# The last 18 tiles of layer 2: two T2 products of three on GpSimd, and every second v = b2|h| + b1 on ScalarE

## The chip, the cores and the metric

The kernel runs on one core of a Trainium2 chip. The metric is the device time of one launch in microseconds (us). The core has a matrix engine (TensorE, PE in the profile), a vector engine (VectorE, DVE), a scalar engine (ScalarE, ACT), a general engine (GpSimd, POOL) and a queue engine (SyncE, SP). Each takes its own instructions in order and waits for the others through semaphores.

## The reference

An attention stage is followed by two layers of the form "tokens times w_in, a function of each element, times w_out". There are 12288 tokens of width 128, and the hidden width is 2048. The function of the second layer is a rational one, and it is the part that the change touches:

```
h  = x @ w_in
P  = a0 + a1*h + a2*h^2 + a3*h^3
Q  = 1 + |b0|*|h| + |b1|*h^2
out = (P / (Q + 1e-6)) @ w_out
```

## The kernel before

**Tiles.** The tokens are cut into 24 chunks of 512 and the hidden width into 16 blocks of 128. One tile is one block of one chunk, 128 x 512 numbers in f32, and there are NB = 384 tiles per layer. The two layers run together in one loop over steps s: step s does tile s of layer 1 and tile t = s - 19 of layer 2 (LAG = 19). Layer 1 ends with s = 383, so that the last tiles of layer 2, from t = 366 on (OFF0 = NB - 18), run with no work of layer 1 beside them. In the text a tile of this stage is named by k = t - 366, from 0 to 17.

**One tile of layer 2.** TensorE writes h into PSUM (`in2`). ScalarE writes u = |h| (L550) and t1 = a3*h + a2 (L551, the scale in a register, the bias from a tile). GpSimd writes v = b2*u + b1 (L404) and w = v*u (L412); here b1 and b2 are the two absolute coefficients in the tile `babs`. T2 = t1*h is made by VectorE (L776, L747), or by GpSimd (L410). GpSimd is given SBUF tiles only, so for a T2 of its own ScalarE first copies h into `hcb` (L557). VectorE makes T3 = (T2 + a1)*h (L770). ScalarE makes ln(1 + w) (L568) and from it r = 1/Q by an exponential (L584), written over h. VectorE makes y = (T3 + a0)*r (L761), the correction e from w and r (L790), and the result g = (e - 2)*y (L785). TensorE adds g times w_out to the sum of the chunk (`out2`, L944 in the last chunk).

**Order.** The order on each engine is written out by hand. In the last stage ScalarE takes for tile t: u, t1, the copy of h if GpSimd makes this T2, then ln and the exponential of tile t-1. GpSimd takes v, T2 if it is its own, and w, all of tile t. VectorE takes y of t-2, T3 of t-1, T2 of t if it is its own, g of t-3, e of t-2. In the last stage TensorE runs three matmuls per tile whose result is not used (L982). When a chunk ends, ScalarE also copies the finished sum out (L514); this happens once in the stage, ahead of tile k = 6. Ahead of tile k = 1 it splits the last chunk's input (L526, L528), and GpSimd makes the low part of it (L397).

**Who makes T2.** `by_pool(t)` says whether GpSimd makes T2 of tile t: of the last 18 tiles every odd k, nine of them; before that, one tile of 16. `pool_t2(t)` counts these tiles. The semaphore `v_rdy` counts the v's.

**The register.** Between the attention stage and the layers ScalarE waits for the last attention sum and loads a3 into a register (L505); after that it takes the first tile of layer 1 (L578, L541). `babs` is written by VectorE (L694).

Of the kernel before, what the change touches and what calls it, by code (L numbers as in the profile page):

```python
# [22 lines left out]
ALU = mybir.AluOpType  # L23
ACT = mybir.ActivationFunctionType
# [6 lines left out]
def build_program(nc, qT, kvT, w_sr, w_in1, w_out1, w_in2, w_out2, coef_a, coef_b, outT):  # L31
# [11 lines left out]
    NF = DFF // P  # L43
    SA = 2 * TPC
    ITERS = NCH // 2
    NB = NCH * NF
# [5 lines left out]
    OFF0 = NB - 18  # L52
    HC_RING = 2
    H1_RING, H2_RING = 2, 4
    U_RING, W_RING, LN_RING, T_RING, R_RING, G_RING = 3, 4, 2, 6, 4, 4
# [11 lines left out]
    with ExitStack() as ctx:  # L67
# [22 lines left out]
        ca, cb, babs = sb("ca", [P, 4], F32), sb("cb", [P, 2], F32), sb("babs", [P, 2], F32)  # L90
# [44 lines left out]
        def sem(name):  # L135
            return ctx.enter_context(nc.semaphore(name))
# [22 lines left out]
        sqh_rdy, sql_rdy = sem("sqh_rdy"), sem("sql_rdy")  # L159
        x2f_rdy, x2l0_rdy = sem("x2f_rdy"), sem("x2l0_rdy")  # L160
        wo1h_rdy, wo1_rdy, g1h_rdy, g1l_rdy = map(sem, ("wo1h_rdy", "wo1_rdy", "g1h_rdy", "g1l_rdy"))
        hc_rdy, t2p_rdy = sem("hc_rdy"), sem("t2p_rdy")
        o_out = [sem("o_out0"), sem("o_out1")]
        wout1_in = sem("wout1_in")
# [4 lines left out]
        def need(eng, s, value):  # L169

            if not isinstance(value, int) or value > 0:
                eng.wait_ge(s, value)
# [58 lines left out]
        T2_COL = 7  # L231

        def by_pool(t):

            return t % 2 == 1 if OFF0 <= t < NB else 0 <= t < OFF0 and t % NF == T2_COL

        POOL_T2 = [t for t in range(NB) if by_pool(t)]

# [48 lines left out]
        def _(pool):  # L287
# [100 lines left out]
            for s in range(STEPS):  # L388
                if s % NF == 5 and 1 <= s // NF < NCH - 1:
                    x1_high(s // NF + 1)  # L390
                    x1_low(s // NF + 1)
                t = s - 3
                if chunk_end(t) and t > NF:
                    c = t // NF
                    pool.wait_ge(x2h_rdy, c + 1)
                    pool.wait_ge(x2f_rdy, c)
                    nc.gpsimd.tensor_tensor(x2l[:, c % 2, :], x2f[:, c % 2, :], x2h[:, c % 2, :].bitcast(F32),  # L397
                                            ALU.subtract).then_inc(x2_rdy, 1)
                t = s - LAG
                if in_b(t):  # L400
                    w = wb[:, t % W_RING, :]
                    u = ub[:, t % U_RING, :]
                    pool.wait_ge(u_rdy, t + 1)
                    nc.gpsimd.tensor_scalar(w, u, babs[:, 1:2], babs[:, 0:1], ALU.mult, ALU.add).then_inc(v_rdy, 1)  # L404
                    if by_pool(t):
                        n = pool_t2(t)
                        p = tb[:, t % T_RING, :]
                        pool.wait_ge(t1_rdy, t + 1)
                        pool.wait_ge(hc_rdy, n + 1)
                        nc.gpsimd.tensor_tensor(p, p, hcb[:, n % HC_RING, :], ALU.mult).then_inc(t2p_rdy, 1)  # L410
                    pool.wait_ge(v_rdy, t + 1)
                    nc.gpsimd.tensor_tensor(w, w, u, ALU.mult).then_inc(w_rdy, 1)  # L412
                t = s
                if in_b(t) and not on_act(t):
                    r = r1[:, t % R_RING, :]
                    pool.wait_ge(r1_rdy, t + 1)
                    need(pool, g1_used, t - G_RING + 1)
                    nc.gpsimd.tensor_tensor(g1[:, t % G_RING, :], r, r, ALU.mult).then_inc(sqp_rdy, 1)  # L418
                    if halved(t):
                        n = halves(t)  # L420
                        pool.wait_ge(sqh_rdy, n + 1)
                        pool.wait_ge(sqp_rdy, squares_pool(t))
                        nc.gpsimd.tensor_tensor(g1l[:, n % 2, :], g1[:, t % G_RING, :], g1h[:, n % 2, :].bitcast(F32),
                                                ALU.subtract).then_inc(sql_rdy, 1)
# [3 lines left out]
        def _(act):  # L428
# [74 lines left out]
            act.wait_ge(coef_in, 32)  # L503
            a3 = act.alloc_register("a3")
            nc.scalar.reg_load(a3, ca[0:1, 3:4].bitcast(mybir.dt.int32))  # L505

            for s in range(STEPS):
                t = s - LAG - 5
                if chunk_end(t):
                    c = t // NF  # L510
                    need(act, o_out[c % 2], c // 2 * 16)
                    if c < NCH - 1:
                        act.wait_ge(g2_used, t + 1)
                        nc.scalar.activation(osb[:, c % 2, :], ACC2, ACT.Copy, scale=-1.0).then_inc(o_rdy, 1)  # L514
                    else:
                        for h in range(2):
                            act.wait_ge(g2_used, 2 * (t + 1) - (NB - NF) - 1 + h)
                            nc.scalar.activation(osb[:, c % 2, h * HT:(h + 1) * HT], ACC_END[h], ACT.Copy,
                                                 scale=-1.0).then_inc(o_rdy, 1)

                t = s - 3
                if chunk_end(t) and t > NF:
                    c = t // NF
                    act.wait_ge(g1_used, t + 1)
                    need(act, h2_rdy, (c - 1) * NF)
                    nc.scalar.activation(x2h[:, c % 2, :], ACC1, ACT.Identity).then_inc(x2h_rdy, 1)  # L526
                    need(act, x2_rdy, c - 2)
                    nc.scalar.activation(x2f[:, c % 2, :], ACC1, ACT.Identity).then_inc(x2f_rdy, 1)  # L528

                t = s - 1  # L530
                if halved(t):
                    n = halves(t)
                    act.wait_ge(r1_rdy, t + 1)
                    need(act, g1_used, t - G_RING + 1)
                    nc.scalar.activation(g1h[:, n % 2, :], r1[:, t % R_RING, :], ACT.Square).then_inc(sqh_rdy, 1)

                t = s - 1
                if in_b(t) and on_act(t) and s != LAG:
                    act.wait_ge(r1_rdy, t + 1)
                    need(act, g1_used, t - G_RING + 1)  # L540
                    nc.scalar.activation(g1[:, t % G_RING, :], r1[:, t % R_RING, :], ACT.Square).then_inc(sqa_rdy, 1)  # L541

                if s == NF + 1:
                    act.wait_ge(g1_used, NF)
                    nc.scalar.activation(x2h[:, 0, :], ACC1, ACT.Identity).then_inc(x2h_rdy, 1)

                t = s - LAG
                if in_b(t):
                    act.wait_ge(h2_rdy, t + 1)
                    nc.scalar.activation(ub[:, t % U_RING, :], h2(t), ACT.Abs).then_inc(u_rdy, 1)  # L550
                    nc.scalar.activation(tb[:, t % T_RING, :], h2(t), ACT.Identity,  # L551
                                         bias=ca[:, 2:3],
                                         scale=a3).then_inc(t1_rdy, 1)
                    if by_pool(t):
                        n = pool_t2(t)
                        need(act, t2p_rdy, n + 1 - HC_RING)
                        nc.scalar.activation(hcb[:, n % HC_RING, :], h2(t), ACT.Identity).then_inc(hc_rdy, 1)  # L557

                t = s - 1
                if in_b(t) and on_act(t) and s == LAG:  # L560
                    act.wait_ge(r1_rdy, t + 1)
                    need(act, g1_used, t - G_RING + 1)
                    nc.scalar.activation(g1[:, t % G_RING, :], r1[:, t % R_RING, :], ACT.Square).then_inc(sqa_rdy, 1)

                t = s - LAG - 1
                if in_b(t):
                    act.wait_ge(w_rdy, t + 1)
                    nc.scalar.activation(lnb[:, t % LN_RING, :], wb[:, t % W_RING, :], ACT.Ln,  # L568
                                         bias=Q_ONE).then_inc(ln_rdy, 1)

                t = s
                if in_b(t):
                    act.wait_ge(h1_rdy, t + 1)
                    if t < NF + R_RING:
                        need(act, g1h_rdy, min(t - R_RING + 1, NF))
                    elif not on_act(t - R_RING):
                        act.wait_ge(sqp_rdy, squares_pool(t - R_RING))
                    nc.scalar.activation(r1[:, t % R_RING, :], H1[t % H1_RING], ACT.Relu).then_inc(r1_rdy, 1)  # L578

                t = s - LAG - 1  # L580
                if in_b(t):
                    act.wait_ge(t3_rdy, t + 1)
                    act.wait_ge(ln_rdy, t + 1)
                    nc.scalar.activation(h2(t), lnb[:, t % LN_RING, :], ACT.Exp,  # L584
                                         scale=-1.0).then_inc(r_rdy, 1)
# [441 lines left out]
```

## Time and profile before

| | |
|---|---|
| median of 3 runs | 1517.66 us (1517.64 to 1517.86) |
| the profiled execution's own time | 1517.89 us |
| its span, first to last instruction | 1515.9 us |
| busy share PE, DVE, ACT, POOL | 98%, 95%, 91%, 82% |
| granted TensorE clock | 1.000 over the span |

The busy shares are means over the whole run. The stage that the change touches is the last 4% of it, from about 1455 us to the end. There, in one slice of 5.62 us after another, the profile repeats the same pair of tiles.

### The profile page before, as it was taken

To read this page: it belongs to the slowest core of one execution; us is meant where nothing else is said; L and a number is where in the kernel's file an instruction comes from. 1 tells how busy PE (TensorE), PEld (TensorE's weight loads), DVE (VectorE), ACT (ScalarE), POOL (GpSimd) and SP (SyncE) were. 2 spreads that over 40 slices of the span, in tenths; PEclk is the share of its full clock that TensorE was granted. 3 is DMA by queue.
4 is the path that set the end of the run, shared out by engine and by line. 5 is a ranking of instruction groups with operands and counts; after the bars stand their busy time and mean duration, and the time that the engine had idled before them with its cause. 6 is when DMAs were issued, how large, how long until landed. Compare 5 with 4: busy or idle time off the path is not lost.

```text
span 1515.9 us, 20584 instructions
## 1 busy us (share of the span) xinstructions
PE 1483.7 (98%) x5576; PEld 991.1 (65%) x5576; DVE 1445.2 (95%) x2549; ACT 1378.8 (91%) x2672; POOL 1248.3 (82%) x1225
## 2 busy tenths in 40 slices
PE   5999999999999999999999999999999999999988
PEld 4999999765666666666666666666666666666655
DVE  7888888889999999999999999999999999999998
ACT  3777777689999999999999999999999999999997
POOL 4544445359999999999999999999999999999897
PEclk9999999999999999999999999999999999999999
DMA  6200001000000000000000000000000000000000
GB/s 224 84 21 28 21 27 43 1 1 1 8 8 8 1 8 8 8 8 1 7 8 8 0 8 8 8 1 8 7 8 1 8 8 8 8 1 8 8 8 7
DMA packets 11518, 24.21 MB, mean 16 GB/s; under 512 B 1440, under 2 KB 2336, under 8 KB 11168
## 3 DMA queue, kind: packets, MB, share of 16 engines
q1 hardware_dynamic: 11424, 23.14, 4.5%
q8 instruction: 36, 0.59, 0.2%
q14 instruction: 58, 0.48, 0.1%
HBM read 16.85 MB, written 6.29 MB: 15 GB/s over the span
## 4 chain that ended last, share of the span: by engine, by line
PE 88%; DVE 5%; ACT 2%; POOL 2%; issue 1%; DMA 1%; SPq 0%; POOLq 0%; ACTq 0%; DVEq 0%
PE psum L937 19%; PE psum L974 18%; PE psum L801 11%; PE psum L800 11%; PE psum L802 11%; PE psum L889 6%; PE psum L852 6%; PE psum L874 4%; DVE tb L727 1%; DVE tb L736 1%; DVE tb L753 1%; DVE g1h L713 1%; DVE psum L741 1%; POOL tb L410 1%; DMA X<-kvT 1%
## 5 line engine op out<-in xcount | busy, mean ns | idle before, releaser
L412 POOL TENSOR_TENSOR wb<-wb,ub 128x512 f32<-128x512 f32 x384 | 496.4, 1293 | 29.4
L937 PE MATMUL psum<-tb,wout 128*128 128x512 f32 x736 | 375.8, 592 | 2.5 <-DVE tb L785 2.3
L974 PE MATMUL psum<-g,wout 128*128 128x512 f32 x690 | 352.4, 592 | 0.2 <-ACT x2f L528 0.2
L404 POOL TENSOR_SCALAR wb<-ub,babs 128x512 f32<-128x512 f32 x384 | 296.0, 771 | 35.5 <-ACT ub L550 30.3
L800 PE MATMUL psum<-x2h,win2h 128*128 128x512 f32 x384 | 283.3, 738 | 2.6 <-POOL x2l L397 2.5
L727 DVE SCALAR_TENSOR_TENSOR tb<-tb,ca,psum 128x512 f32<-128x512 f32 x364 | 267.8, 736 | 4.6 <-ACT psum L584 4.5
L736 DVE SCALAR_TENSOR_TENSOR tb<-tb,ca,psum 128x512 f32<-128x512 f32 x365 | 269.6, 739 | 0.0
L551 ACT ACTIVATE tb<-psum,ca 128x512 f32<-128x512 f32 x384 | 267.1, 696 | 0.0
L550 ACT ACTIVATE ub<-psum 128x512 f32<-128x512 f32 x384 | 233.0, 607 | 23.5 <-PE psum L802 23.5
L568 ACT ACTIVATE lnb<-wb 128x512 f32<-128x512 f32 x384 | 248.3, 647 | 5.2 <-POOL wb L412 4.8
L753 DVE SCALAR_TENSOR_TENSOR tb<-psum,tb 128x512 f32<-128x512 f32 x364 | 248.1, 682 | 2.6
L741 DVE SCALAR_TENSOR_TENSOR psum<-wb,psum 128x512 f32<-128x512 f32 x364 | 249.5, 685 | 0.0
L584 ACT ACTIVATE psum<-lnb 128x512 f32<-128x512 f32 x384 | 240.1, 625 | 2.6 <-DVE tb L770 0.6
L974 PEld LDWEIGHTS psum<-g,wout 128*128 128x128 f32 x690 | 130.9, 190 | 163.7 <-issue 162.0
L578 ACT ACTIVATE r<-psum 128x512 f32<-128x512 f32 x384 | 234.9, 612 | 2.4 <-PE psum L802 0.3
L747 DVE TENSOR_TENSOR tb<-tb,psum 128x512 f32<-128x512 f32 x343 | 232.5, 678 | 4.0 <-ACT tb L551 4.0
L418 POOL TENSOR_TENSOR g<-r 128x512 f32<-128x512 f32 x184 | 191.9, 1043 | 33.2 <-ACT r L578 33.2
L334 POOL TENSOR_SCALAR pnorm<-prob,stat 128x768 f32<-128x768 f32 x96 | 87.3, 909 | 127.8 <-DVE stat L637 122.0
L937 PEld LDWEIGHTS psum<-tb,wout 128*128 128x128 f32 x736 | 138.4, 188 | 36.4 <-DVE tb L785 3.8
L801 PE MATMUL psum<-x1l,win1h 128*128 128x512 f32 x384 | 153.0, 398 | 0.0
L801 PE MATMUL psum<-x2l,win2h 128*128 128x512 f32 x384 | 152.9, 398 | 0.0
L800 PE MATMUL psum<-x1h,win1h 128*128 128x512 f32 x384 | 151.9, 396 | 0.0
(109 smaller groups left out, 2506.6 us busy)
## 6 DMA issues: line engine op xcount, KB each, us to landing
qraw<-qT SPq DMA_DIRECT2D x23, 256.0 KB, 2.6
outT<-osb SPq DMA_DIRECT2D x23, 256.0 KB, 2.0
X<-kvT SPq DMA_DIRECT2D x15, 384.0 KB, 7.7
wraw<-w_in SPq DMA_DIRECT2D x2, 1024.0 KB, 8.3
X<-kvT SPq DMA_DIRECT2D x2, 192.0 KB, 10.5
outT<-osb SPq DMA_DIRECT2D x2, 128.0 KB, 1.8
qraw<-qT SPq DMA_DIRECT2D x1, 192.0 KB, 10.2
wsr<-w_sr SPq DMA_DIRECT2D x1, 64.0 KB, 1.8
```

The source lines that it names most:

```text
L404: nc.gpsimd.tensor_scalar(w, u, babs[:, 1:2], babs[:, 0:1], ALU.mult, ALU.add).then_inc(v_rdy, 1)
L412: nc.gpsimd.tensor_tensor(w, w, u, ALU.mult).then_inc(w_rdy, 1)
L551: nc.scalar.activation(tb[:, t % T_RING, :], h2(t), ACT.Identity, bias=ca[:, 2:3], scale=a3).then_inc(t1_rdy, 1)
L568: nc.scalar.activation(lnb[:, t % LN_RING, :], wb[:, t % W_RING, :], ACT.Ln, bias=Q_ONE).then_inc(ln_rdy, 1)
L727: nc.vector.scalar_tensor_tensor(out=y, in0=y, scalar=ca[:, 0:1], in1=r, op0=ALU.add, op1=ALU.mult).then_inc(y_rdy, 1)
L736: nc.vector.scalar_tensor_tensor(out=p, in0=p, scalar=ca[:, 1:2], in1=h2(t), op0=ALU.add, op1=ALU.mult).then_inc(t3_rdy, 1)
L741: nc.vector.scalar_tensor_tensor(out=r, in0=wb[:, t % W_RING, :], scalar=Q_ONE, in1=r, op0=ALU.add, op1=ALU.mult).then_inc(e_rdy, 1)
L753: nc.vector.scalar_tensor_tensor(out=y, in0=h2(t), scalar=-2.0, in1=y, op0=ALU.add, op1=ALU.mult).then_inc(g2_rdy, 1)
L800: mm(out, lh, rh, start=start, stop=False)
L801: mm(out, lh, rl, start=False, stop=False)
L937: mm(ACC2, wout2[:, f, :], tb[:, t % T_RING, :], start=(f == 0), stop=(f == NF - 1))\
L974: mm(ACC1, wout1[:, f, :], g1[:, t % G_RING, :], start=(f == 0), stop=(f == NF - 1))\
```

## The change

Three things change, all within the last 18 tiles but for one register load. T2 is made by GpSimd for k = 1, 2, 4, 5, 7, 8, and so on, 12 tiles in place of 9. For every odd k, v is made by ScalarE (an Identity activation with scale b2 in a register and bias b1 from `babs`), right behind t1 and ahead of the copy of h; GpSimd's w then waits for that. And ScalarE loads b2 into a register beside a3, with a wait for `babs`.

```
         def by_pool(t):
-            return t % 2 == 1 if OFF0 <= t < NB else 0 <= t < OFF0 and t % NF == T2_COL
+            return (t - OFF0) % 3 > 0 if OFF0 <= t < NB else 0 <= t < OFF0 and t % NF == T2_COL
+        def v_on_act(t):
+            return OFF0 <= t < NB and (t - OFF0) % 2 == 1
+        def v_acts(t):
+            return sum(v_on_act(x) for x in range(t))
 ...  (GpSimd)
-                    pool.wait_ge(u_rdy, t + 1)
-                    nc.gpsimd.tensor_scalar(w, u, babs[:, 1:2], babs[:, 0:1], ALU.mult, ALU.add).then_inc(v_rdy, 1)
+                    if not v_on_act(t):
+                        pool.wait_ge(u_rdy, t + 1)
+                        nc.gpsimd.tensor_scalar(w, u, babs[:, 1:2], babs[:, 0:1], ALU.mult, ALU.add).then_inc(v_rdy, 1)
                     if by_pool(t):
                         ... T2 on GpSimd, unchanged
-                    pool.wait_ge(v_rdy, t + 1)
+                    if v_on_act(t):
+                        pool.wait_ge(va_rdy, v_acts(t) + 1)
+                    else:
+                        pool.wait_ge(v_rdy, t + 1 - v_acts(t))
                     nc.gpsimd.tensor_tensor(w, w, u, ALU.mult).then_inc(w_rdy, 1)
 ...  (ScalarE, before the loop)
+            act.wait_ge(babs_rdy, 1)
+            b2 = act.alloc_register("b2")
+            nc.scalar.reg_load(b2, babs[0:1, 1:2].bitcast(mybir.dt.int32))
 ...  (ScalarE, behind t1)
+                    if v_on_act(t):
+                        act.wait_ge(u_rdy, t + 1)
+                        need(act, e_rdy, t + 1 - W_RING)
+                        nc.scalar.activation(wb[:, t % W_RING, :], ub[:, t % U_RING, :], ACT.Identity,
+                                             bias=babs[:, 0:1], scale=b2).then_inc(va_rdy, 1)
```

## Rows read from the trace of the kernel before

**Rows 1.** Busy time in one pair of tiles: stretch, us, busy (x count) by engine, clock, DMA.
```profile
1486.93:1492.55 5.62, 5.04 (x21) 3.61 (x21) 5.62 (x10) 5.03 (x11) 5.32 (x6) 1.00 0.00 0
```

**Rows 2.** Chain that ended last, in one pair: start us, us, what.
```profile
1483.09 1.29 POOL tb L410
1484.38 1.26 POOL wb L412
...
1485.66 0.64 ACT lnb L568
```

**Rows 3.** Timeline of ScalarE, k = 9 and 10: start us, us, engine line op, [idle before].
```profile
1481.30 0.58 ACT L550 ACTIVATE ub<-psum 128x512 f32<-128x512 f32 x1
1481.78 0.68 ACT L551 ACTIVATE tb<-psum,ca 128x512 f32<-128x512 f32 x1
1482.35 0.60 ACT L557 ACTIVATE hcb<-psum 128x512 f32<-128x512 f32 x1
1482.82 0.64 ACT L568 ACTIVATE lnb<-wb 128x512 f32<-128x512 f32 x1
1483.56 0.60 ACT L584 ACTIVATE psum<-lnb 128x512 f32<-128x512 f32 x1
1484.09 0.58 ACT L550 ACTIVATE ub<-psum 128x512 f32<-128x512 f32 x1
1484.57 0.68 ACT L551 ACTIVATE tb<-psum,ca 128x512 f32<-128x512 f32 x1
1485.66 0.63 ACT L568 ACTIVATE lnb<-wb 128x512 f32<-128x512 f32 x1 [0.41 <-POOL wb L412]
```

**Rows 4.** Timeline of GpSimd, k = 1, then k = 9 and 10.
```profile
1459.50 0.78 POOL L404 TENSOR_SCALAR wb<-ub,babs 128x512 f32<-128x512 f32 x1
1460.23 1.29 POOL L410 TENSOR_TENSOR tb<-tb,hcb 128x512 f32<-128x512 f32 x1
...
1483.09 1.29 POOL L410 TENSOR_TENSOR tb<-tb,hcb 128x512 f32<-128x512 f32 x1 [0.23 <-ACT hcb L557]
1484.34 1.29 POOL L412 TENSOR_TENSOR wb<-wb,ub 128x512 f32<-128x512 f32 x1
1485.61 0.77 POOL L404 TENSOR_SCALAR wb<-ub,babs 128x512 f32<-128x512 f32 x1
1486.47 1.27 POOL L412 TENSOR_TENSOR wb<-wb,ub 128x512 f32<-128x512 f32 x1
```

**Rows 5.** Timeline of VectorE, T2 and g of k = 10 and 7.
```profile
1485.52 0.68 DVE L776 TENSOR_TENSOR tb<-tb,psum 128x512 f32<-128x512 f32 x1
1486.11 0.68 DVE L785 SCALAR_TENSOR_TENSOR tb<-psum,tb 128x512 f32<-128x512 f32 x1
```

**Rows 6.** Timeline of ScalarE, a square from SBUF to SBUF.
```profile
1442.02 0.64 ACT L541 ACTIVATE g<-r 128x512 f32<-128x512 f32 x1
1442.55 0.60 ACT L550 ACTIVATE ub<-psum 128x512 f32<-128x512 f32 x1
```

**Rows 7.** The line of the register load: duration ns min/median/max, first and last start us.
```profile
L505 ACTq TENSOR_LOAD <-ca x1: 465/465/465, 293.3 to 293.3; - x1
```

**Rows 8.** Timeline where layer 1 begins.
```profile
293.90 0.60 ACT L578 ACTIVATE r<-psum 128x512 f32<-128x512 f32 x1
...
296.10 0.47 PE L800 MATMUL psum<-g1h,wo1h 128*128 128x512 f32 x1 [0.59 <-DVE g1l L716]
```

**Rows 9.** Timeline of ScalarE: u of k = 1, copy out, u of k = 7 and 17, last ln.
```profile
1457.99 0.60 ACT L550 ACTIVATE ub<-psum 128x512 f32<-128x512 f32 x1
...
1472.46 0.58 ACT L514 ACTIVATE osb<-psum 128x512 f32<-128x512 f32 x1
...
1475.66 0.60 ACT L550 ACTIVATE ub<-psum 128x512 f32<-128x512 f32 x1 [0.32 <-PE psum L802]
...
1503.78 0.58 ACT L550 ACTIVATE ub<-psum 128x512 f32<-128x512 f32 x1
...
1508.12 0.63 ACT L568 ACTIVATE lnb<-wb 128x512 f32<-128x512 f32 x1 [1.49 <-POOL wb L412]
```

More of the change, by code:

```diff
@@ L161, in build_program @@
         wo1h_rdy, wo1_rdy, g1h_rdy, g1l_rdy = map(sem, ("wo1h_rdy", "wo1_rdy", "g1h_rdy", "g1l_rdy"))
+        va_rdy = sem("va_rdy")
         hc_rdy, t2p_rdy = sem("hc_rdy"), sem("t2p_rdy")
```

## The prediction, made before the result was known

> **What bounds the stage now.** I looked first at the busy time by stretches, because the shares of the page are means over a run in which the change touches only the last 60 us. In one pair of tiles (5.62 us) VectorE is busy all 5.62, GpSimd 5.32, ScalarE 5.03 and TensorE 5.04 [rows 1]. That says VectorE, but the shares hide how near the others are. So I read the chain of waits next, and it doesn't run through VectorE: it goes from GpSimd's T2 to w to ScalarE's ln [rows 2], and from there along ScalarE to the next copy of h. The reader is to see in the timelines that this loop closes. From ScalarE's copy of h to GpSimd's T2 is 1483.09 - 1482.35 = 0.74; from T2 to w 1.25; from w to ln 1485.66 - 1484.34 = 1.32 [rows 3, 4]. On ScalarE, start to start, u takes 0.48, t1 0.57, the copy 0.475, ln 0.73 (the exponential needs its result) and the exponential 0.54 [rows 3]. The loop is 0.74 + 1.25 + 1.32 + 0.73 + 0.54 + 0.48 + 0.57 = 5.63 per pair, which is what the pair takes. VectorE's work happens to be as long: two limits lie on each other, and a third is close. ScalarE's own work in a pair is 2 x 2.32 + 0.475 = 5.12, with 0.52 free (the trace shows 0.41 as idle, the rest is the tail of t1) [rows 3]. GpSimd's own free time is the 0.23 before its T2 [rows 4]. An edit here must be read as a loop over all engines.
>
> **What the change takes away.** VectorE loses 3 T2 of 0.60 each, start to start (1486.11 - 1485.52) [rows 5]: per six tiles its work goes from 3 x 5.62 = 16.9 to 16.3. GpSimd loses nine v and gains three T2: per six tiles it has 3 x 0.86 for v with w behind it or 0.73 with T2 behind it, 4 x 1.25 and 6 x 1.27, at most 15.2 instead of 16.9 [rows 4]. Both have room then, some 2.7 and 2.5 per tile.
>
> **What it adds, and where.** Everything else lands on ScalarE: nine v and three more copies of h. The copy is 0.475 [rows 3]. The v isn't in the trace. It reads SBUF and writes SBUF, as the square does, which takes 0.54 from start to start [rows 6]; and it has a bias from a tile and a scale in a register, as t1 has, which takes 0.57 where the plain copy from the same place takes 0.475 [rows 3]. So I take 0.54 + 0.09 = 0.63. Bounds: 0.475 below, as cheap as the copy, and 0.73 above, the spacing of ln, the longest that any activation of this stage shows [rows 3]. Its wait for u costs nothing: u ends 0.58 after its start, and v could start at 1.05 anyway. Its wait for e of tile t-4 is long over. What is queued behind v is the copy of h and with it GpSimd's T2 and w, so a late v delays both.
>
> The page "ScalarE: Activation LUTs" of the Trainium skill, section "What ACT_TABLE_LOAD costs", gives an activation with a pointer bias as 280 ns plus 0.833 ns per element, with neighbours overlapping by 93 ns; an estimate from it is 0.61 for v, and with it the sum below would be about 0.1 lower. No run here has shown v yet, but t1 in the trace, 0.68 busy, is a little under the 0.71 of that rule.
>
> The Trainium skill's page "GPSIMD Engine Reference", section "Engine selection", says that a product of two tiles belongs on VectorE, as GpSimd is about twice as slow with two inputs. The trace agrees (1.29 against 0.68), and going by this rule alone the three moved T2 would lose 3 x (1.25 - 0.60) = 2.0 us. By the loop they cost something else, which is worked out next.
>
> **The new cycle.** The pattern repeats every six tiles. I go along ScalarE's queue from one u to the next. A plain tile is 0.48 + 0.57 + 0.73 + 0.54 = 2.32; the copy adds 0.475, v adds 0.63.
> - k = 1, 5 (both): 2.32 + 0.475 + 0.63 = 3.43.
> - k = 4 (copy): 2.80.
> - k = 2 (copy): 2.80 of its own. Ln of k = 1 can't start before 0.74 + 1.25 + 1.32 = 3.31 after the copy of k = 1, and ScalarE arrives at 0.475 + 0.73 + 0.54 + 0.48 + 0.57 + 0.475 = 3.27: a stall of 0.04, so 2.83.
> - k = 3 (v): 2.95 of its own. GpSimd was still with w of k = 1 when u of k = 2 was there, so for k = 2 v, T2 and w come behind each other: from the copy of k = 1, T2 at 0.74, w at 1.99, v of k = 2 at 3.25, T2 at 3.98, w at 5.23, ln at 6.55. ScalarE arrives at 3.31 + 0.73 + 0.54 + 0.48 + 0.57 + 0.63 = 6.26. A stall of 0.29: 3.24.
> - k = 0 (nothing): 2.32 of its own, but ln of k = 5 needs 3.31 from the copy of k = 5 and ScalarE arrives at 2.80: 2.83.
>
> Together 2 x 3.43 + 2.80 + 2.83 + 3.24 + 2.83 = 18.56 for six tiles, against 3 x 5.62 = 16.87 before: +1.69, or 0.28 per tile. Of this 0.85 is ScalarE's own work beyond the old cycle (17.71 against 16.87), and the rest are three stalls in which GpSimd is late. VectorE needs 16.3 and waits. So the limit moves from a loop over GpSimd to ScalarE's queue, and the three T2 taken from VectorE buy nothing.
>
> **The whole stage.** k = 0 is untouched. From u of k = 1 at 1457.99 [rows 9] the steps 3.43, 2.83, 3.24, 2.80 and 3.43 bring ScalarE to the copy out at 1473.72 instead of 1472.46. From there TensorE sets the next distance: u of k = 7 waited for it and came 3.20 after the copy out [rows 9], so it comes at 1476.92 instead of 1475.66, +1.26 (the copy out and this wait hide the stall of k = 6). From k = 7 to 17 are ten steps: 3.43 + 2.83 + 3.24 + 2.80 + 3.43 + 2.83 + 3.43 + 2.83 + 3.24 + 2.80 = 30.86, before 1503.78 - 1475.66 = 28.12: +2.74. For k = 17, from u to the last ln, there are 0.48 + 0.57 + 0.63 + 0.74 + 1.25 + 1.32 = 4.99 instead of 4.34 [rows 9]: +0.65. What follows the last ln is the same. Sum 1.26 + 2.74 + 0.65 = 4.65 us.
>
> **The second register.** Loading a3 took 0.465 [rows 7], from 293.3 to 293.77, and the first tile of layer 1 started at 293.90, when TensorE's result was there: the first load is hidden. A second one behind it ends at about 294.27. Nothing covers it: VectorE waits for that tile, and TensorE waits 0.59 for VectorE [rows 8]; the chain of waits stays on this pair through the whole first chunk. The wait for `babs` itself is over. I take +0.45; bounds 0 (if TensorE or VectorE makes it up) and 0.55 (a load, a wait and a little dispatch).
>
> **Sum.** 1517.89 is the profiled execution's own time; 1517.89 + 4.65 + 0.45 = 1522.99. It stands 0.23 above the median of the runs, so I predict 1522.8. Six of the nine v count fully (those of k = 3, 9, 15 lie before a stall), so the bounds of v give 6 x (0.475 - 0.63) = -0.9 and 6 x (0.73 - 0.63) = +0.6; with the register the likeliest case spans 1521.4 to 1523.5.
>
> **Rivals.**
> - *Only ScalarE's work counts.* If GpSimd, with less to do on average, caught up wherever I see a stall, six tiles would take 17.71: +0.85 per six, 2.4 over the 17 tiles, with the register +2.8: 1520.5. For it: GpSimd has 1.7 us less work per six tiles. Against: the stalls come from latency (copy, T2, w, ln in line), not from load, and the 0.41 idle in front of ln [rows 3] is the same thing today. 9%.
> - *VectorE is the true limit, and the edit is a gain.* If the loop only looks closed and ScalarE's instructions can be packed tighter behind each other than they stand now, the time follows VectorE: -3 x 0.60, and +0.45: 1516.3. For it: VectorE's 5.62 of 5.62 [rows 1]. It decides where ScalarE's added work per pair, 0.63 + 0.16 for a third of a copy, fits into its free 0.52: v and the share of the copy would have to be under 0.52, thus v under 0.36. The shortest activation of this size in the rows is 0.475 apart. 4%.
> - *The T2 pairs fall out worse.* GpSimd's v of k = 2 waits for w, and if T2 behind it took 0.86 instead of 0.73 to follow, the stall of k = 3 grows by 0.13 and the total by 0.4; if v also came at its upper bound, 1523.9. 8%.
> - *The forecast:* 79%.
>
> **Chances.** What a measurement of this kernel can tell from no change is about 0.2%, 3.0 us: below 1514.6, or above 1520.7. The forecast and the third rival lie above; the first rival lies just inside. Faster 0.04, same 0.10, slower 0.86. The range reaches down to the first rival and up past the third: 1520.4 to 1524.3.
>
> **What would show it.** In the profile after: v as an activation of about 0.72 us, followed by the next after 0.63; a cycle of 18.56 us for six tiles, with ScalarE busy nearly throughout and idle only ahead of ln of k = 5, 11 (0.4 as the profile counts it) and of k = 2, 8, 14; VectorE waiting for the exponential where it had no gap; GpSimd no longer in the chain except at those places; two register loads, and the first tile of layer 1 at about 294.35. I am wrong if the cycle is under 17.7, if VectorE has no idle time, or if v takes under 0.5.

## The result

| | changed kernel | before |
|---|---|---|
| median of 7 runs each | 1522.77 us (1522.46 to 1524.05) | 1517.86 us (1517.64 to 1518.38) |
| the profiled execution's own time, span | 1522.46, 1520.5 | 1517.89, 1515.9 |

The ratio is 1.0034, with a 95% interval of 1.0023 to 1.0046: slower by 4.9 us, where 1522.8 was forecast. The runs of the changed kernel lie in two groups, four from 1522.46 to 1522.77 and three from 1523.66 to 1524.05. The forecast had the first group and not the second, and the median falls into the first by one run.

The page of the changed kernel shows where the work went. ScalarE has 12 activations more (2672 before), VectorE 3 and GpSimd 6 instructions less:

```profile
span 1520.5 us, 20600 instructions
...
PE 1485.9 (98%) x5576; PEld 992.3 (65%) x5576; DVE 1444.4 (95%) x2546; ACT 1385.4 (91%) x2684; POOL 1245.1 (82%) x1219
```

The busy time by stretches of the changed kernel (us, then TensorE, weight loads, VectorE, ScalarE, GpSimd, clock, DMA) has one cycle of six tiles, from u of k = 9 to u of k = 15, in its last row. It answers to the pair in [rows 1]:

```profile
1459.00:1460.00 1.00, 0.21 (x1) 0.21 (x2) 1.00 (x3) 1.00 (x3) 0.74 (x1) 0.98 0.00 0
1460.00:1462.00 2.00, 2.00 (x5) 1.21 (x5) 0.68 (x2) 1.91 (x4) 1.38 (x2) 0.50 0.03 8
1462.00:1464.00 2.00, 2.00 (x6) 1.11 (x5) 2.00 (x4) 1.91 (x5) 2.00 (x3) 0.66 0.00 0
...
1483.29:1501.77 18.48, 15.16 (x62) 10.85 (x61) 16.75 (x26) 17.30 (x33) 14.87 (x14) 1.00 0.00 0
```

Six tiles take 18.48 us in place of 16.87. VectorE, which had no gap, is free for 1.73 us of them and GpSimd for 3.61. ScalarE is now the busiest, with 1.18 us free in six tiles, 0.62 of it ahead of the two ln that wait for w (k = 8 and 11).

The first three rows show something else. TensorE has waited for x2l, the low part of the last chunk's input, and behind this wait its granted clock is 0.50 (1.2 GHz) for over 3 us. In the trace of before the same wait is as long and the clock behind it is 1.00. The timelines of TensorE, first in the changed kernel and then in the kernel before:

```profile
1459.79 0.67 PE L821 MATMUL psum<-x2h,win2h 128*128 128x512 f32 x1 [2.19 <-POOL x2l L406]
...
1474.49 1.13 PE L965 MATMUL psum<-tb,wout 128*128 128x256 f32 x4 [2.14 <-ACT osb L530]
```

```profile
1459.57 0.50 PE L800 MATMUL psum<-x2h,win2h 128*128 128x512 f32 x1 [2.19 <-POOL x2l L397]
...
1473.10 1.13 PE L944 MATMUL psum<-tb,wout 128*128 128x256 f32 x4 [0.98 <-ACT osb L514]
```

The second row of each is the wait for the copy out, which grew from 0.98 to 2.14 us: ScalarE reaches the copy out 1.40 us later than before. Behind it the clock is 1.00 in both of these executions (1474 to 1478 us).

ScalarE's timeline shows the stretches that the prediction walked through: the first tile of layer 1; u of k = 1; the copy out; u of k = 7 and 9; v of k = 9 and the ln behind it; u of k = 11, and the v and the copy of h with it; the ln of that tile; u of k = 15 and 17; the last ln.

```profile
294.12 0.60 ACT L599 ACTIVATE r<-psum 128x512 f32<-128x512 f32 x1 [0.31 <-PE psum L823]
...
1458.21 0.60 ACT L566 ACTIVATE ub<-psum 128x512 f32<-128x512 f32 x1
...
1473.86 0.58 ACT L530 ACTIVATE osb<-psum 128x512 f32<-128x512 f32 x1
...
1477.05 0.60 ACT L566 ACTIVATE ub<-psum 128x512 f32<-128x512 f32 x1 [0.34 <-PE psum L823]
...
1483.29 0.58 ACT L566 ACTIVATE ub<-psum 128x512 f32<-128x512 f32 x1
...
1484.34 0.72 ACT L573 ACTIVATE wb<-ub,babs 128x512 f32<-128x512 f32 x1
1485.28 0.63 ACT L589 ACTIVATE lnb<-wb 128x512 f32<-128x512 f32 x1 [0.22 <-POOL wb L425]
...
1489.33 0.58 ACT L566 ACTIVATE ub<-psum 128x512 f32<-128x512 f32 x1
...
1490.38 0.72 ACT L573 ACTIVATE wb<-ub,babs 128x512 f32<-128x512 f32 x1
1490.99 0.59 ACT L578 ACTIVATE hcb<-psum 128x512 f32<-128x512 f32 x1
...
1494.29 0.63 ACT L589 ACTIVATE lnb<-wb 128x512 f32<-128x512 f32 x1 [0.40 <-POOL wb L425]
...
1501.77 0.58 ACT L566 ACTIVATE ub<-psum 128x512 f32<-128x512 f32 x1
...
1507.82 0.58 ACT L566 ACTIVATE ub<-psum 128x512 f32<-128x512 f32 x1
...
1512.75 0.63 ACT L589 ACTIVATE lnb<-wb 128x512 f32<-128x512 f32 x1 [1.47 <-POOL wb L425]
```

Who waited for whom from 1480 to 1509 us (us, times, longest): VectorE's y for the exponential, seven times, and ScalarE's ln for w only three times.

```profile
DVE tb L782 <- ACT psum L605: 2.7, 7, 0.8
...
ACT lnb L589 <- POOL wb L425: 0.8, 3, 0.4
```

The second register load is in the trace, shorter than the first (ns, start us):

```profile
L518 ACTq TENSOR_LOAD <-ca x1: 457/457/457, 293.3 to 293.3; - x1
...
L521 ACTq TENSOR_LOAD <-babs x1: 278/278/278, 293.8 to 293.8; - x1
```

The profile puts the 0.31 of idle time ahead of the first tile (294.12) down to TensorE. But the matmul that it names was over at about 293.88, and the second load ran until about 294.1, so the tile more likely waited for the load:

```profile
293.49 0.39 PE L823 MATMUL psum<-x1h,win1l 128*128 128x512 f32 x1
```

### The profile page after: what moved, and what is told of

It reads as the page before. It is cut to its first block, busy times and chain, and to the rows that moved or that the text cites. A ratio compares the mean times of both kernels' runs of the same rounds, so it can differ in the third digit from the quotient of the medians.

```text
span 1520.5 us, 20600 instructions
## 1 busy us (share of the span) xinstructions
PE 1485.9 (98%) x5576; PEld 992.3 (65%) x5576; DVE 1444.4 (95%) x2546; ACT 1385.4 (91%) x2684; POOL 1245.1 (82%) x1219
## 2 busy tenths in 40 slices
DMA packets 11518, 24.21 MB, mean 16 GB/s; under 512 B 1440, under 2 KB 2336, under 8 KB 11168
## 4 chain that ended last, share of the span: by engine, by line
PE 88%; DVE 5%; ACT 3%; POOL 2%; issue 1%; DMA 0%; SPq 0%; POOLq 0%; ACTq 0%; DVEq 0%
PE psum L958 19%; PE psum L995 18%; PE psum L822 11%; PE psum L821 11%; PE psum L823 11%; PE psum L910 6%; PE psum L873 6%; PE psum L895 4%; DVE tb L748 1%; DVE tb L757 1%; DVE tb L774 1%; DVE g1h L734 1%; DVE psum L762 1%; POOL tb L420 1%; POOL wb L425 1%
## 5 line engine op out<-in xcount | busy, mean ns | idle before, releaser
L414 POOL TENSOR_SCALAR wb<-ub,babs 128x512 f32<-128x512 f32 x375 | 289.1, 771 | 37.3 <-ACT ub L566 32.5
```

## The experiments

All were run beside the kernel before on the same chip; its median there was 1517.87, 1517.90 and 1517.81 us in the three sets of four. In what was written ahead of them, "loops and queues" is the prediction's way of counting: each engine in its order, each wait with its latency.

| kernel | median (lowest to highest), us | against before | runs |
|---|---|---|---|
| reg_only | 1517.80 (1517.39 to 1518.22) | -0.1 | 11 |
| t2_only | 1520.29 (1520.00 to 1522.01) | +2.4 | 11 |
| v_only | 1523.19 (1523.08 to 1523.48) | +5.3 | 5 |
| v_late | 1521.59 (1520.60 to 1522.22) | +3.7 | 10 |
| reg_early | 1523.49 (1522.23 to 1524.46) | +5.6 | 5 |
| gap_filled | 1524.43 (1522.85 to 1524.66) | +6.5 | 5 |
| v_even | 1518.77 (1518.41 to 1519.30) | +0.9 | 11 |
| t2_trim | 1518.16 (1517.41 to 1518.61) | +0.3 | 11 |
| after_filled | 1523.27 (1523.02 to 1523.42) | +5.5 | 5 |
| before_filled | 1518.04 (1517.79 to 1518.40) | +0.2 | 11 |
| t2_skip1 | 1517.31 (1517.01 to 1517.73) | -0.5 | 11 |
| skip1_filled | 1518.16 (1517.50 to 1518.45) | +0.4 | 11 |

**One part at a time: t2_only.** The kernel before with only this line:

```
-            return t % 2 == 1 if OFF0 <= t < NB else ...
+            return (t - OFF0) % 3 > 0 if OFF0 <= t < NB else ...
```

> Only the 12 T2 on GpSimd, every v stays there. Theory A (loop through GpSimd): three tiles need at least 0.86 + 2 x 0.73 for v, 2 x 1.25 for T2 and 3 x 1.27 for w = 8.6 us on GpSimd alone, and some 8.8 with the wait for the copy, against 8.44 before: the stage is 2.2 us longer. Theory B (VectorE is the limit): 3 x 0.60 = 1.8 us shorter.

+2.4 us, theory A. GpSimd's timeline from v of k = 9 to v of k = 12 shows three tiles in 1494.08 - 1485.23 = 8.85 us, where 8.8 was expected, with one wait of 0.22:

```profile
1485.23 0.76 POOL L404 TENSOR_SCALAR wb<-ub,babs 128x512 f32<-128x512 f32 x1
...
1488.32 1.27 POOL L410 TENSOR_TENSOR tb<-tb,hcb 128x512 f32<-128x512 f32 x1 [0.22 <-ACT hcb L557]
...
1491.56 1.29 POOL L410 TENSOR_TENSOR tb<-tb,hcb 128x512 f32<-128x512 f32 x1
1492.80 1.31 POOL L412 TENSOR_TENSOR wb<-wb,ub 128x512 f32<-128x512 f32 x1
1494.08 0.78 POOL L404 TENSOR_SCALAR wb<-ub,babs 128x512 f32<-128x512 f32 x1
```

Three T2 taken from VectorE save nothing, although VectorE was busy all the time. In this kernel the loop's limit is GpSimd itself, whose own work is 8.6 of the 8.85. Four of its eleven runs, 1521.3 to 1522.0, stand apart from the rest, as in the changed kernel. The profiled execution (1521.52) is one of these four. In it TensorE waits for the copy out, the clock behind this wait is 0.71 from 1474 to 1476 us and 0.50 from 1476 to 1478, and ScalarE waits for h of k = 7. The rows of TensorE's and of ScalarE's timeline:

```profile
1473.87 1.17 PE L944 MATMUL psum<-tb,wout 128*128 128x256 f32 x4 [1.84 <-ACT osb L514]
```

```profile
1477.64 0.60 ACT L550 ACTIVATE ub<-psum 128x512 f32<-128x512 f32 x1 [1.11 <-PE psum L802]
```

**The other part: v_only.** The changed kernel with the old `by_pool`.

```
-            return (t - OFF0) % 3 > 0 if OFF0 <= t < NB else ...
+            return t % 2 == 1 if OFF0 <= t < NB else ...
```

> T2 stays at every odd k; v of every odd k is on ScalarE, ahead of the copy of h, with the register. Theory A (the v stands in the loop copy, T2, w, ln, exponential, u, t1): the pair takes 5.63 + 0.61 = 6.24 us, the stage is 5.0 longer, with the register +5.2, so more than the whole change. Theory B (ScalarE's work counts alone): the pair takes 5.12 + 0.61 = 5.73, the stage is 1.0 longer, with the register +1.2.

+5.3 us, theory A: one half of the change alone costs more than the whole. ScalarE's timeline in this kernel, from one ln that waits for w to the next:

```profile
1482.69 0.63 ACT L589 ACTIVATE lnb<-wb 128x512 f32<-128x512 f32 x1 [0.40 <-POOL wb L425]
...
1484.99 0.73 ACT L573 ACTIVATE wb<-ub,babs 128x512 f32<-128x512 f32 x1
1485.61 0.60 ACT L578 ACTIVATE hcb<-psum 128x512 f32<-128x512 f32 x1
...
1488.91 0.63 ACT L589 ACTIVATE lnb<-wb 128x512 f32<-128x512 f32 x1 [0.40 <-POOL wb L425]
```

The pair takes 6.22 us, the loop's 5.63 and v's 0.61, and the 0.40 of idle time in front of ln is where it was before: ScalarE isn't full, v simply stands in the loop. A low clock has a small share in the +5.3: from 1466 to 1468 us it is 0.50 in this trace, ScalarE waits 0.65 for h there, and that pair takes 6.45.

**The same instructions in other places: v_late and v_even.** In v_late the whole change stands, with the two blocks swapped:

```
+                    if by_pool(t):
+                        n = pool_t2(t)
+                        need(act, t2p_rdy, n + 1 - HC_RING)
+                        nc.scalar.activation(hcb[:, n % HC_RING, :], h2(t), ACT.Identity).then_inc(hc_rdy, 1)
                     if v_on_act(t):
...
-                    if by_pool(t):
...
```

> The whole change, but v is issued behind the copy of h and not ahead of it. No instruction is added or removed. Theory A: the v leaves the path copy, T2, w, and is done before w needs it; tiles with both cost what ScalarE needs, the stalls shrink: 2.1 us less than the change, +2.4 to +2.6 against the kernel before. Theory B (only the sum of ScalarE's work counts): no difference from the change, +4.6 to +5.

Its ten runs lie in two groups, four from 1520.60 to 1520.81 and six from 1521.46 to 1522.22. The lower one is 2.8 us above before and some 1.9 below the lower group of the change; expected were 2.4 to 2.6 and 2.1. The upper group, 1521.77 in the middle, is 1.9 below the upper group of the change (1523.70). The median of all ten, +3.7, falls into the upper group and is above what was expected. So order alone takes about two of the five microseconds. The busy time by stretches says what is left: ScalarE is busy 19.44 of 20 us.

```profile
1480.00:1500.00 20.00, 16.88 (x68) 11.93 (x66) 18.65 (x30) 19.44 (x36) 17.20 (x16) 1.00 0.00 0
```

v_even keeps the old T2 and makes v on ScalarE for k = 2, 4, 6 and so on (eight tiles), which have no copy of h:

```
-            return (t - OFF0) % 3 > 0 if OFF0 <= t < NB else ...
+            return t % 2 == 1 if OFF0 <= t < NB else ...
...
-            return OFF0 <= t < NB and (t - OFF0) % 2 == 1
+            return OFF0 < t < NB and (t - OFF0) % 2 == 0
```

> T2 stays at every odd k; v goes to ScalarE for the even k, which have no copy of h. Theory A (loops and queues): from the copy of an odd tile ScalarE needs 0.475 + 0.73 + 0.54 + 0.48 + 0.57 + 0.61 = 3.41 to the ln that GpSimd lets go after 3.31, so v fills the 0.50 in which ScalarE stood idle: 5.73 per pair, 0.9 us more over the stage, with the register +1.1. Against v at the odd tiles (+5.3 measured) the place of the same instruction decides over 4 us. Theory B (nine v on ScalarE cost the same wherever they stand): +5.

+0.9 us, theory A. In ScalarE's timeline v of k = 10 fills what was the stall: the ln behind it has no idle time, and the pair takes 1487.84 - 1482.13 = 5.71.

```profile
1482.13 0.58 ACT L566 ACTIVATE ub<-psum 128x512 f32<-128x512 f32 x1
...
1485.97 0.72 ACT L573 ACTIVATE wb<-ub,babs 128x512 f32<-128x512 f32 x1
1486.59 0.62 ACT L589 ACTIVATE lnb<-wb 128x512 f32<-128x512 f32 x1
...
1487.84 0.58 ACT L566 ACTIVATE ub<-psum 128x512 f32<-128x512 f32 x1
```

Eight v here cost 0.9 us, nine at the odd tiles 5.3. The 0.9 by itself isn't clear of the scatter (the interval of the ratio is 0.9997 to 1.0015), but the +5 of theory B is excluded.

**The register: reg_only and reg_early.** reg_only adds the wait and the load to the kernel before.

```
             nc.scalar.reg_load(a3, ca[0:1, 3:4].bitcast(mybir.dt.int32))
+            act.wait_ge(babs_rdy, 1)
+            b2 = act.alloc_register("b2")
+            nc.scalar.reg_load(b2, babs[0:1, 1:2].bitcast(mybir.dt.int32))
```

> Only the second register load (with its wait for babs) is added to the kernel before. Theory A (queue order and latency decide): its trace shows the first tile of layer 1 0.22 us later and all behind it with it, so +0.2 us, and the TensorE clock stays at 1.00 in every run, as it does before. Theory B (the prediction's own size): +0.45. Theory C (the shift of the start is what makes the TensorE clock drop behind the wait for x2l, seen in the changed kernel): most runs below clock 1.000, and some of them 1.2 us longer.

It measures less than it meant to: its trace has one register load, that of a3. Nothing uses b2 in this kernel and the program came out without the load, so only the wait can have run, and it has no cost that the runs resolve (the interval is 0.9991 to 1.0009). So neither the +0.2 nor the +0.45 was tested by this run, and theory C wasn't either. reg_early has both loads ahead of the last attention copy:

```
-            for j in range(TAIL_A):
+            for j in range(TAIL_A - 1):
                 step_a(ITERS, j)
-            act.wait_ge(pv_rdy, NCH)
-            act.wait_ge(ql_rdy, NCH)
             act.wait_ge(coef_in, 32)
             a3 = act.alloc_register("a3")
 ...  (both loads, unchanged)
+            step_a(ITERS, TAIL_A - 1)
+            act.wait_ge(pv_rdy, NCH)
+            act.wait_ge(ql_rdy, NCH)
```

> The whole change, but both register loads stand ahead of ScalarE's last attention copy, where it waits for TensorE anyway. Theory A (the second load, 0.278 us in the trace, delays the first tile of layer 1 by 0.20): that tile comes 0.70 after the copy again, as before, and the time is 0.2 us below the change's. Theory B (something else of the new program moved the start): no difference.

The loads now run at 288.6 and 289.1 us. The first tile of layer 1 comes 0.78 after the copy, with TensorE named as what it waited for; in the changed kernel it came 0.90 after it, before 0.70. Theory A expected 0.70, so 0.12 of the 0.20 came back. The lowest runs are 1522.23 and 1522.75, against 1522.46 for the change, so what this gives in the time lies within the scatter of the runs, and three of five are in the upper group. In the profiled execution, one of these three (1523.50), the place of the loss can be seen. TensorE's timeline, ScalarE's timeline and the stretches:

```profile
1474.19 1.30 PE L966 MATMUL psum<-tb,wout 128*128 128x256 f32 x4 [2.14 <-ACT osb L531]
...
1476.56 0.63 PE L822 MATMUL psum<-x2h,win2h 128*128 128x512 f32 x1
```

```profile
1478.08 0.60 ACT L567 ACTIVATE ub<-psum 128x512 f32<-128x512 f32 x1 [1.67 <-PE psum L824]
```

```profile
1474.00:1476.00 2.00, 1.81 (x6) 1.56 (x7) 1.83 (x4) 1.91 (x5) 1.92 (x3) 0.75 0.35 131
1476.00:1478.00 2.00, 2.00 (x6) 1.54 (x6) 2.00 (x4) 0.41 (x1) 1.17 (x1) 0.50 0.00 0
```

TensorE has stood for 2.14 us waiting for the copy out, the clock falls to 1.2 GHz, and the matmuls of h take 0.63 in place of 0.39. Just there, at k = 7, ScalarE waits for h: 1.67 us in place of the 0.34 of the changed kernel's profiled execution. That is 1.3 us, about the distance between the groups. In that other execution the clock fell at 1460 us, where ScalarE didn't wait for h, and it is one of the lower group.

**TensorE kept busy: gap_filled, after_filled, before_filled.** gap_filled is the changed kernel with 8 matmuls whose result isn't used:

```
+            def fill_gap():
+                pe.wait_ge(r1_rdy, NB)
+                for _ in range(8):
+                    mm(H1[1], win1h[:, 0:P], x1h[:, 0, :], start=True, stop=True)
 ...
+                if s == NB + 2:
+                    fill_gap()
```

> The whole change, and 8 matmuls whose result is not used are put on TensorE where it stands idle for 2.19 us waiting for x2l. Theory A (this idle time is what lets the TensorE clock fall to half, in a part of the runs, and costs up to 1.3 us there): the clock is 1.00 around 1460 us, and all runs lie together near 1522.5. Theory B (the clock falls because TensorE has more idle time in the whole stage): the runs still lie in two groups 1.2 us apart.

Theory A as written is refuted. The wait for x2l shrank from 2.19 to 0.34 (the eight stand one tile early and held up u of k = 1 by 0.31 too), but the low clock came later instead, in two places of the profiled execution, and three runs are at 1524.4 or above:

```profile
1464.00:1466.00 2.00, 2.00 (x5) 1.11 (x5) 1.80 (x3) 1.93 (x4) 2.00 (x3) 0.67 0.00 0
1466.00:1468.00 2.00, 2.00 (x6) 1.57 (x5) 1.96 (x5) 1.67 (x4) 1.80 (x2) 0.50 0.00 0
1474.00:1476.00 2.00, 1.21 (x3) 1.03 (x4) 1.57 (x3) 2.00 (x5) 2.00 (x3) 0.73 0.20 75
1476.00:1478.00 2.00, 2.00 (x6) 1.54 (x6) 2.00 (x4) 0.92 (x2) 1.69 (x2) 0.50 0.15 56
```

The first of these falls stands behind another wait of TensorE, 1.90 for VectorE's g:

```profile
1463.96 1.38 PE L958 MATMUL psum<-tb,wout 128*128 128x512 f32 x2 [1.90 <-DVE tb L806]
```

The second one stands behind the copy out again, after 2.20 us of waiting, and ScalarE waits 1.96 for h of k = 7. It isn't one gap, then. after_filled fills the stage: the same 8, 4 ahead of the first sum of the last chunk, and 4 per tile in place of 3, from two tiles earlier on. before_filled is the kernel before with the same edit.

```
-    WARM, WARM_B = 4, 3
+    WARM, WARM_B = 4, 4
...
+                if s == NB + 2:
+                    fill_gap(8)
...
+                    if s - LAG - 4 == NB - NF:
+                        fill_gap(4)
                     out2(s - LAG - 4)
-                    if NB + 4 <= s < STEPS - 4:
+                    if NB + 2 <= s < STEPS - 4:
```

> The whole change, with TensorE kept busier over the whole stage by matmuls whose result is not used: 8 in the wait for x2l, 4 ahead of the first sum of the last chunk, and 4 per tile in place of 3, from k = 1 on. Theory A (the upper group of the changed kernel's runs, 1.2 us above the lower, comes from stretches at half clock, and these from TensorE's idle time in the stage): the clock is 1.000 in nearly every run and all lie near 1522.5. Theory B (the idle time doesn't matter): two groups again. If the added matmuls hold up the real ones, all runs lie above 1522.8.

All five runs have a clock of 1.000 and lie within 0.4 us, with no second group. The two other kernels with this fill, further down, have 22 runs at 1.000. This bears theory A out, in its wider form: with TensorE's idle time filled the clock doesn't fall, and the second group is gone. The expectation that all runs would lie near 1522.5 failed. The fill has its price, and all runs lie some 0.7 above the change's lower group, so the median is no better than that of the change: u of k = 1 comes 0.31 late and u of k = 7 waits 0.58 instead of 0.34. Its busy time from 1440 to 1480 us, against 34.66 of 40 at a clock of 0.96 in the changed kernel:

```profile
1440.00:1480.00 40.00, 37.71 (x133) 24.39 (x132) 36.79 (x59) 37.41 (x69) 32.74 (x30) 1.00 0.02 8
```

**Where the upper group loses its time.** TensorE's wait for the copy out differs between the kernels. In the profiled executions it is 2.14 us in the change, 1.95 in v_late, 1.84 in t2_only, 2.14 in reg_early and 2.20 in gap_filled; the runs of these five spread over 1.6 to 2.2 us. It is 1.29 in v_only, 1.05 in v_even and 0.99 in after_filled, whose runs spread over 0.4 to 0.9. The spread alone is weak evidence: the kernel before, with a wait of 0.98, spreads over 1.0 to 1.8 us in its 21 to 27 runs. The traces say more. Three of the five were profiled in a slower run (t2_only, reg_early, gap_filled): in all three the clock falls right behind this wait, and from u of k = 6 to u of k = 7 ScalarE takes 3.92, 4.05 and 4.33 us. Two were profiled in a run of the lower group (the change, v_late): there the clock stays at 1.00 behind it, and the same distance is 2.71 and 2.72. So the loss of 1.2 to 1.6 us is seen at one place in three traces. That the total of TensorE's idle time decides isn't borne out: the change has it busy for 23.99 of the 30 us from 1480 on, and v_only for 23.97, and no trace shows a fall there. Which of the filled waits matters was not separated.

> The kernel before with the same fill of TensorE. Theory A: its runs above 1518.2 go, the median falls by 0 to 0.3 us. Theory B: TensorE has 2.74 us of work per tile at 2.81 us per tile then, so the added matmuls hold up h of the next tile, and the time grows by 0.3 to 1.

+0.2 us, eleven runs all at clock 1.000 within 0.6 us; the kernel before spreads over 1.5 us in the same set, five of its 27 runs at a clock of 0.998 or at 1518.3 and above. Theory A expected the runs above 1518.2 to go; four of eleven still lie there (1518.30 to 1518.40), and the measured +0.2 lies between the two theories. The median doesn't gain: the fill costs about what the clock gives.

**Fewer T2 on GpSimd: t2_trim, t2_skip1, skip1_filled.** All three change one line of the kernel before:

```
-            return t % 2 == 1 if OFF0 <= t < NB else ...
t2_trim:
+            return t - OFF0 in (3, 5, 7, 9, 11, 13, 14) if OFF0 <= t < NB else ...
t2_skip1, skip1_filled:
+            return t % 2 == 1 and t > OFF0 + 1 if OFF0 <= t < NB else ...
```

> The kernel before, with T2 on GpSimd at k = 3, 5, 7, 9, 11, 13 and 14 only; no v on ScalarE, no second register. Theory A (loops and queues): without k = 1 the copy of h and the late GpSimd no longer delay the start (0.7 less), and without k = 15 and 17 the last tile doesn't wait for T2, w behind each other (1.4 less): 2.2 us faster than the kernel before. Theory B (VectorE is the limit and gets two T2 more): 1.2 us slower.

A miss: +0.3 where -2.2 was expected. The expected gain at the end counted only ScalarE's and GpSimd's path to the last exponential and forgot that this waits for VectorE's T3. With two T2 more, VectorE is late there: the stretch of the last tiles shows it busy 10.69 of 10.72 us, and the last exponential waits 1.96 for it. From u of k = 17 to the last y it takes 6.53 us in place of 5.70, so the end is 0.8 worse and not 1.4 better. Of the 0.7 at the start the profiled execution shows only 0.11 (17.56 us from u of k = 1 to u of k = 7, before 17.67). There is a low clock there, 0.71 in the first row, and ScalarE waits 0.90 for h of k = 3:

```profile
1458.17:1464.12 5.95, 4.36 (x9) 2.27 (x10) 5.73 (x10) 4.63 (x10) 5.34 (x5) 0.71 0.01 4
1500.85:1511.57 10.72, 7.92 (x31) 5.55 (x31) 10.69 (x19) 6.18 (x11) 5.45 (x6) 1.00 0.00 0
```

```profile
1509.24 0.60 ACT L584 ACTIVATE psum<-lnb 128x512 f32<-128x512 f32 x1 [1.96 <-DVE tb L770]
```

> The kernel before, with T2 of k = 1 alone given back to VectorE. Theory A (loops and queues): VectorE waited 0.72 for the exponential at k = 2, so it has room there, and the late copy, T2, w no longer stall ln by 0.82: 0.7 us faster than before. Theory B (VectorE is the limit over the whole stage): 0.6 us slower.

-0.5 us in the medians, 1517.31 against 1517.81, where -0.7 was expected. All eleven of its runs lie below the median of before, but the interval of the ratio, 0.9988 to 1.0006, holds 1, so that it beats the kernel before is likely and not shown. The 0.82 in front of ln is gone, as expected, but the profiled execution (1517.41) has another wait in its place. The clock is 0.50 from 1460 to 1462 us, behind the wait for x2l, and ScalarE waits for h of k = 2:

```profile
1461.05 0.60 ACT L550 ACTIVATE ub<-psum 128x512 f32<-128x512 f32 x1 [0.87 <-PE psum L802]
```

> T2 of k = 1 given back to VectorE, and the fill of TensorE. Theory A: 0.7 us faster than the kernel before, with no run at a low clock. Theory B: as before_filled, the fill costs what the other edit gains.

This one also has the fill of before_filled. +0.4 us: theory B, the fill takes more than the other edit gives, at a clock of 1.000 throughout. On this kernel the fill costs 0.85 us (1518.16 against 1517.31), on the kernel before 0.2.

## Why the prediction was right, and where it was lucky

| step | predicted | in the trace of the changed kernel |
|---|---|---|
| v, from start to next start | 0.63 | 0.61 (1490.38 to 1490.99, k = 11) |
| six tiles, k = 9 to 15 | 18.56 | 18.48 |
| idle ahead of ln of k = 11 | 0.4 | 0.40 |
| u of k = 1 to u of k = 7 | 18.93, +1.26 | 18.84, +1.17 |
| u of k = 7 to u of k = 17 | 30.86, +2.74 | 30.77, +2.65 |
| u of k = 17 to last ln | 4.99, +0.65 | 4.93, +0.59 |
| stage in all | +4.65 | +4.41 |
| register load | +0.45 | +0.20 |

**The mechanism held.** The reading that mattered was that the loop of copy, T2, w, ln, exponential, u and t1 adds up to the pair's 5.63 us, so that whatever is put into that loop counts in full, and VectorE's 100% did not mean that relieving VectorE helps. t2_only and v_only bear it out from two sides, and v_late and v_even with the same instructions elsewhere. The idle times came where they were forecast, ahead of ln of k = 2, 8 and 14 (0.21, 0.22, 0.23) and of k = 11 (0.40); only that of k = 5 isn't there, hidden by the copy out as the prediction's own walk had said. The effects of the parts don't add: +2.4 and +5.3 alone, +4.9 together. A likely reason is that v on ScalarE frees GpSimd, which was what t2_only lacked; no run isolates it.

**The rivals.** "Only ScalarE's work counts" is refuted by v_only (6.22 per pair where the work alone is 5.73), and holds nearly for v_late, where v doesn't delay the copy of h: six tiles from u of k = 7 take 17.62 there, and the work alone is 17.71 by the prediction. "VectorE is the limit" is refuted for the change, where VectorE is free for 1.73 us in six tiles. It is right for the last tiles of t2_trim, but not wherever VectorE gets work: t2_skip1 gives it a T2 at a place where it waited, and isn't slower. "T2 pairs fall out worse" didn't occur: tile k = 9 takes 3.25, where the forecast had 3.24 and this rival 3.37.

**The mis-sized term** is the register load. The step said "a second one behind it ends at about 294.27", with the first load's 0.465. The second took 0.278, and the tile started at 294.12: +0.22 by the clock, +0.20 from the copy ahead of it. The stage was 0.24 too large, of which 0.12 is v (six times 0.02). By the trace the sum is 1517.89 + 4.41 + 0.20 = 1522.50, and the profiled execution is at 1522.46. That the load's 0.20 reaches the end of the program is read from the trace; no run isolates it.

**The missing term** is the clock. The prediction let ScalarE come to the copy out 1.26 us later and didn't ask what TensorE does meanwhile. TensorE waits for it, 2.14 us in place of 0.98. In the traces of three related kernels the clock falls behind this wait and h of k = 7 comes 1.2 to 1.6 us later, which is the distance between the groups. For the change itself no execution of the upper group was profiled, so that its three slower runs lost their time there is inferred. What decides in which run the clock falls stays open: the same waits stand in traces without a fall.

**The luck.** Both steps that can be compared were forecast too large, the stage by 0.24 and the register by 0.25. Against that, the runs lie in two groups, which lifts their median above the profiled execution by 0.31, and the median of before rose from 1517.66 to 1517.86 with more runs. The mechanism forecast +5.1 and +4.9 was measured, a good hit; that 1522.8 meets 1522.77 within 0.03 is luck. Three runs of seven were 1.2 us above the others; had one more been, the median would have been near 1523.7, still in the range but 0.9 above the forecast.

## What to carry to other kernels

Where an engine is busy all the time, check whether a loop over the others is just as long before you relieve it; add the latencies along the loop, and ask of each added instruction whether it stands in it. The same v cost 0.1 us per tile outside the loop and 0.6 inside. And where a change makes TensorE wait longer at one place, its clock may fall behind that wait in some of the runs, so look at the granted clock around its longest waits, and at how the runs are spread, not only at the median.

## What was not expected of the hardware

- TensorE's granted clock fell to 0.50 (1.2 GHz) for 3 to 4 us at a time in a stretch in which TensorE was busy 87% (34.66 of 40 us). In the traces looked at, the falls stand behind waits of 1.8 to 2.2 us: for x2l (the change, v_late, t2_skip1, t2_trim), for VectorE's g (v_only, gap_filled) or for the copy out (t2_only, reg_early, gap_filled). Such waits stand without a fall, too: the kernel before waits 2.19 for x2l, and the changed kernel 2.14 for the copy out, both at 1.00 behind it.
- A fall at 1460 us cost nothing in the changed kernel, while in t2_skip1 ScalarE waited 0.87 for h there. At 1475 us it cost 1.2 to 1.6 us in three traces.
- Two register loads behind each other took 0.457 to 0.465 and 0.278 us: the second was cheaper in all six traces in which both were looked up (the change, v_only, v_late, v_even, gap_filled, and reg_early at 289.1 us).
